# Fetching the expert marks at the start of a round and splitting the gate chain around the w2 splits in a fused attention, mixture-of-experts and dense kernel

## The reference

```python
def _moe_ref(x, expert_emb, tau, w1, w2):
    N, D = x.shape                                   # 4608, 512
    xn = x / (np.linalg.norm(x, axis=-1, keepdims=True) + 1e-06)
    en = expert_emb / (np.linalg.norm(expert_emb, axis=-1, keepdims=True) + 1e-06)
    logits = xn @ en.T / tau
    expert_idx = np.argmax(logits, axis=1)
    logits_shift = logits - logits.max(-1, keepdims=True)
    probs = np.exp(logits_shift)
    probs /= probs.sum(-1, keepdims=True) + 1e-09
    gate_w = probs[np.arange(N), expert_idx]
    for e in range(E):                               # E = 8
        mask = expert_idx == e
        h = np.maximum(x[mask] @ w1[e], 0.0)         # w1: 512 x 1024
        out[mask] = gate_w[mask, None] * (h @ w2[e]) # w2: 1024 x 512
    return out

def _moe2_ref(x, w_in, w_out, s, b):
    h = x @ w_in                                     # 512 x 2048
    g = s * np.maximum(h, 0.0) ** 2 + b
    return g @ w_out                                 # 2048 x 512
```

## Time and profile before

| What | Value |
|---|---|
| Median of three executions | 1391.1 us (1390.35 to 1391.83) |
| The profiled execution, its own time | 1393.17 us |
| Its span, first to last instruction | 1391.1 us |
| TensorE busy | 1345.2 us, 97% of the span |
| VectorE busy | 645.1 us, 46% |
| ScalarE busy | 506.7 us, 36% |
| GpSimd busy | 192.6 us, 14% |
| Mean granted TensorE clock | 0.993 of full speed |

### The profile page before, as it was taken

How to read it: one execution, slowest core, us unless ns; L and a number is a source line. 1 busy time by engine, 2 the same in 40 slices (tenths; PEclk the granted TensorE clock), 3 DMA queues, 4 the chain that set the end, 5 groups by cost and what they waited for, 6 DMA issues and landing times.

```text
span 1391.1 us, 23074 instructions
## 1 busy us (share of the span) xinstructions
PE 1345.2 (97%) x6908; PEld 1105.3 (79%) x6909; DVE 645.1 (46%) x1648; ACT 506.7 (36%) x951; POOL 192.6 (14%) x341
## 2 busy tenths in 40 slices
PE   7998899999999999999999999999999999999996
PEld 5776688877788778779888888888888888888884
DVE  5898546666645664757323223232232332322322
ACT  4885335545434643544222222222222222222221
POOL 2236322221222122200001001000010010100101
PEclk9999999999999999999999999999999999999998
DMA  8755313553512451240100001001010010100000
GB/s 252 224 145 193 115 57 103 180 184 108 184 49 68 149 185 49 71 170 9 48 0 31 32 0 62 0 15 47 0 62 0 0 62 0 62 0 0 31 0 31
DMA packets 71938, 103.61 MB, mean 74 GB/s; under 512 B 40424, under 2 KB 41048, under 8 KB 70624
## 3 DMA queue, kind: packets, MB, share of 16 engines
q1 hardware_dynamic: 57824, 72.16, 15.8%
q0 software_dynamic: 8448, 20.40, 4.4%
q10 hardware_dynamic: 5632, 10.60, 2.0%
HBM read 71.81 MB, written 31.34 MB: 74 GB/s over the span
## 4 chain that ended last, share of the span: by engine, by line
PE 81%; DVE 7%; issue 4%; DMA 2%; DVEq 2%; POOL 1%; ACT 1%; ACTq 0%; POOLq 0%; SPq 0%
PE bank_a L1570 26%; PE bank_n L1589 14%; PE bank_tt L1589 12%; PE bank_a L1492 11%; PE bank_n L1525 10%; DMA xg<-x_tok,g_idx 2%; PE bank_tt L1505 1%; PE bank_n L1423 1%; DVEq L363 1%; POOL slot_tab L497 1%; PE bank_tt L1294 1%; PE bank_a L1275 1%; DVE w_in_lo L1044 1%; DVEq L366 1%; PE bank_l L1556 1%
## 5 line engine op out<-in xcount | busy, mean ns | idle before, releaser
L1212 DVE TENSOR_TENSOR sq<-rel 128x512 f32<-128x512 f32 (+1 forms) x144 | 95.4, 663 | 478.4 <-ACT rel L817 478.4
L817 ACT ACTIVATE rel<-bank_a 128x512 f32<-128x512 f32 (+1 forms) x144 | 82.8, 575 | 534.9 <-PE bank_a L1570 534.9
L1570 PE MATMUL bank_a<-y_hi,w_in_hi 128*128 128x512 f32 (+1 forms) x576 | 218.1, 379 | 1.5 <-DVE y_lo L1204 1.4
L1570 PE MATMUL bank_a<-y_hi,w_in_lo 128*128 128x512 f32 (+1 forms) x576 | 217.6, 378 | 0.0
L1570 PE MATMUL bank_a<-y_lo,w_in_hi 128*128 128x512 f32 (+1 forms) x576 | 217.6, 378 | 0.0
L582 POOL DMA_INDIRECT out_rows<-w_raw,out_id x34 | 32.9, 968 | 714.5 <-DVE w_raw L1223 652.1
L1570 PEld LDWEIGHTS bank_a<-y_hi,w_in_hi 128*128 128x128 f32 x576 | 108.4, 188 | 23.0 <-DVE y_lo L1204 1.8
L1570 PEld LDWEIGHTS bank_a<-y_lo,w_in_hi 128*128 128x128 f32 x576 | 108.4, 188 | 20.6 <-issue 0.2
L1570 PEld LDWEIGHTS bank_a<-y_hi,w_in_lo 128*128 128x128 f32 x576 | 108.4, 188 | 19.9
L1525 PE MATMUL bank_n<-w_hi,hid_hi 128*128 128x512 f32 x296 | 115.5, 390 | 1.5 <-DVE hid_lo L1069 1.5
L1525 PE MATMUL bank_n<-w_hi,hid_lo 128*128 128x512 f32 x296 | 115.4, 390 | 0.0
(11 more groups left out here) (237 smaller groups left out, 2136.3 us busy)
## 6 DMA issues: line engine op xcount, KB each, us to landing
w_raw<-in_moe_w SPq DMA_DIRECT2D x16, 2048.0 KB, 10.6
moe_tok<-yg ACTq DMA_DIRECT2D x38, 272.0 KB, 2.1
x_tok<-x_rows SPq DMA_DIRECT2D x8, 1088.0 KB
y_rows<-moe_tok SPq DMA_DIRECT2D x8, 1088.0 KB, 5.3
x_m<-in_x SPq DMA_DIRECT2D x7, 1024.0 KB, 9.4
win_raw<-in_moe_w_in SPq DMA_DIRECT2D x8, 512.0 KB, 10.7
w_raw<-in_moe_w_out SPq DMA_DIRECT2D x1, 4096.0 KB, 16.2
slot_tab<-w_lo SPq DMA_DIRECT2D x2, 1152.0 KB, 6.6
```

What stands on the lines that cost most here:

```text
L817: nc.scalar.activation(rel[:, k, 0:cols], ps_g[k][:, 0:cols], ACT.Relu).then_inc(rel_ready, 1)
L1212: nc.vector.tensor_tensor(sq[:, 0:cols], rel[:, k, 0:cols], rel[:, k, 0:cols], ALU.mult).then_inc(sq_ready, 1)
L1570: last = nc.tensor.matmul(ps_g[n % 2][:, 0:cols], w[:, wc], a[:, c, 0:cols], start=(c == 0 and w is w_in_hi and a is y_hi), stop=(c == DC ...
```

## The change

The table gets one more entry, the last tile less one, and each engine reads it. In a round, VectorE and ScalarE read the marks of tiles g and g+1 (ScalarE the output row too) at the round's start, and `next_w1`, `next_w2` and `store` take them as arguments. On VectorE, `gate_scale` is cut into `gate_norm` (8 steps) and `gate_root` (9 steps), with `next_w2` between them. On ScalarE, `next_w2` comes before `store`. The loop ends one round earlier on TensorE, VectorE, ScalarE and GpSimd, and the last round is written out with only the work that the last tile needs.

```diff
@@ gpsimd
-            with pool.Fori(2, last) as g:
+            with pool.Fori(2, prev) as g:
                 gather(g + 3)
                 result_ids(g)
+            result_ids(prev)
             result_ids(last)
@@ scalar
-            def store(g):
+            def store(g, row=None):
+                row = rows_of(act, g) if row is None else row
                 act.wait_ge(yg_ready, g + 1)
                 act.wait_ge(yid_done, g + 2)
-                act.dma_start(moe_tok[ds(rows_of(act, g), P), :], yg[:]).then_inc(moe_stored, 16)
+                act.dma_start(moe_tok[ds(row, P), :], yg[:]).then_inc(moe_stored, 16)
...
             def tile(g):
+                e, changes = experts(g)
+                e_next, changes_next = experts(g + 1)
+                row = rows_of(act, g)
                 hidden(g + 1)
                 x_hi(g + 2)
                 gate_square(g + 3)
-                next_w1(g + 1)
+                next_w1(e_next, changes_next)
                 gate_soft(g + 1)
                 result(g)
                 hidden_hi(g + 1)
-                store(g)
-                next_w2(g)
-
-            with act.Fori(2, last) as g:
+                next_w2(e, changes, e_next)
+                store(g, row)
+
+            with act.Fori(2, prev) as g:
                 tile(g)
+            hidden(last)
+            gate_soft(last)
+            result(prev)
+            hidden_hi(last)
+            e_a, c_a = experts(prev)
+            e_b, _ = experts(last)
+            next_w2(e_a, c_a, e_b)
+            store(prev)
@@ vector
+            def experts(g):
+                return expert_of(dve, g), changes_after(dve, g)
...
+            def gate_norm(g):
+                n_gate, gate_link = gate_linker(g, 0)
                 dve.wait_ge(gate_lg, g + 1)
...
+                rsqrt_seed(gate_link, gc[:, 0:1], gc[:, 4:5].bitcast(i32), gi[:, 0:1])
+                rsqrt_rounds(gate_link, gc[:, 4:5], gc[:, 5:6], gc[:, 0:1], 1)
+                assert n_gate[0] == NORM_STEPS
+
+            def gate_root(g):
+                n_gate, gate_link = gate_linker(g, NORM_STEPS)
+                rsqrt_rounds(gate_link, gc[:, 4:5], gc[:, 5:6], gc[:, 0:1], 2)
                 gate_link(nc.vector.tensor_tensor(gc[:, 6:7], gc[:, 0:1], gc[:, 4:5], ALU.mult))
                 gate_link(nc.vector.tensor_scalar(gc[:, 6:7], gc[:, 6:7], NORM_EPS, None, ALU.add))
                 nc.vector.reciprocal(gc[:, 1:2], gc[:, 6:7]).then_inc(gate_in, 1)
...
             def tile(g):
+                e, changes = experts(g)
+                e_next, changes_next = experts(g + 1)
                 x_lo(g + 2)
                 gate_logits(g + 3)
-                next_w1(g + 1)
+                next_w1(e_next, changes_next)
                 gate_final(g + 1)
                 hidden_lo(g + 1)
-                gate_scale(g + 2)
-                next_w2(g)
-
-            with dve.Fori(2, last) as g:
+                gate_norm(g + 2)
+                dve.sem_inc(norm_turn, 1)
+                next_w2(e, changes, e_next)
+                gate_root(g + 2)
+
+            with dve.Fori(2, prev) as g:
                 tile(g)
+            gate_final(last)
+            hidden_lo(last)
+            e_a, c_a = experts(prev)
+            e_b, _ = experts(last)
+            next_w2(e_a, c_a, e_b)
@@ tensor
-            with pe.Fori(2, last_g) as g:
+            prev = tile_ahead_of_last(pe)
+            with pe.Fori(2, prev) as g:
                 tile(g)
+            turn_hidden(prev)
+            up(last_g)
+            down(prev)
             turn_hidden(last_g)
```

More of the change, by code:

```diff
@@ L86, in attention_moe_ffn @@
         emb_t = sb(top, "emb_t", [P, PAIRS, E], f32)
-        tile_tab = sb(top, "tile_tab", [P, 3 * NSLOT + 1], i32)
+        tile_tab = sb(top, "tile_tab", [P, 3 * NSLOT + 2], i32)
         slot_w = sb(top, "slot_w", [P, IDW], f32)
@@ L99, in attention_moe_ffn @@
         gi = sb(top, "gi", [P, 2], i32)
-        used = sum(-(-n // 32) * 32 for n in (4 * P, 4 * P, 2 * P, 2 * P, 4 * PAIRS * E, 4 * (3 * NSLOT + 1), 4 * IDW, 4, 4 * NSLOT, 4 * NSLOT,
+        used = sum(-(-n // 32) * 32 for n in (4 * P, 4 * P, 2 * P, 2 * P, 4 * PAIRS * E, 4 * (3 * NSLOT + 2), 4 * IDW, 4, 4 * NSLOT, 4 * NSLOT,
                                               4, 4, 4, 4 * TROWS, 4 * E, 4 * E, 32, 8))
@@ L163, in attention_moe_ffn @@
         tab_f = sb(am, "tab_f", [P, 4, NSLOT], f32)
-        tab_o = sb(am, "tab_o", [P, 3 * NSLOT + 1], f32)
+        tab_o = sb(am, "tab_o", [P, 3 * NSLOT + 2], f32)
         o_slot = sb(am, "o_slot", [P, NSLOT], f32)
@@ L177, in attention_moe_ffn @@
             4 * COLS, 2 * COLS * E, 4 * E, 2 * (B + 1) * E, 4 * COLS, 4 * B * COLS, 4 * COLS * E, 4 * COLS * E, 4 * B * COLS * IDW,
[L178 removed]
+            4 * NSLOT, 8 * E, 48 * E, 4 * NSLOT * E, 4 * NSLOT * E, 16 * NSLOT, 4 * (3 * NSLOT + 2), 4 * NSLOT, 4, 4 * NSLOT, 16, 4 * E,
             4 * E, 4 * NSLOT, 4 * NSLOT * E, 4 * NSLOT, 4 * RW))
@@ L316, in attention_moe_ffn @@
         gate_in = sem("gate_in")
+        norm_turn = sem("norm_turn")
         gate_exp = sem("gate_exp")
@@ L347, in attention_moe_ffn @@
         GATE_STEPS = 17
+        NORM_STEPS = 8
         O_C = TROWS - HEAD
@@ L360, in last_tile, with tile_ahead_of_last @@
             return eng.value_load(tile_tab[0:1, 3 * NSLOT:3 * NSLOT + 1], min_val=E - 1 + EARLY - 1, max_val=MAXT - 1)
+        def tile_ahead_of_last(eng):
+            return eng.value_load(tile_tab[0:1, 3 * NSLOT + 1:3 * NSLOT + 2], min_val=E - 1 + EARLY - 2, max_val=MAXT - 2)
         def expert_of(eng, g):
@@ L443, in _ @@
             sp.sem_inc(load_turn, 1)
-            sp.wait_ge(gate_sq, last + 3)
+            sp.wait_ge(gate_sq, last + 2)
             sp.sem_inc(load_turn, 1)
@@ L548, in _ @@
             last = last_tile(pool)
+            prev = tile_ahead_of_last(pool)
             def result_ids(g):
@@ L701, in win_hi, with next_w1 @@
                 nc.scalar.activation(w_in_hi[:, ds(e * SLOT, SLOT)], win_raw[:], ACT.Copy).then_inc(win_hi_done, 1)
-            def next_w1(g):
-                e = expert_of(act, g)
-                with act.If(changes_after(act, g) > 0):
+            def experts(g):
+                return expert_of(act, g), changes_after(act, g)
+            def next_w1(e, changes):
+                with act.If(changes > 0):
                     act.wait_ge(w1_loaded, 16 * e + 32)
@@ L709, in next_w1, with next_w2 @@
                         nc.scalar.activation(w1_hi[:, c], w_raw[:, c], ACT.Copy).then_inc(w1_hi_done, 1)
-            def next_w2(g):
-                e = expert_of(act, g)
-                with act.If(changes_after(act, g) > 0):
+            def next_w2(e, changes, e_next):
+                with act.If(changes > 0):
                     act.wait_ge(w2_loaded, 16 * e + 32)
@@ L717, in next_w2 @@
                                              w_raw[:, WCOLS + k * SLOT:WCOLS + (k + 1) * SLOT], ACT.Copy).then_inc(w2_hi_done, 1)
-                    win_hi(expert_of(act, g + 1))
+                    win_hi(e_next)
             def hidden_hi(g):
@@ L759, in _ @@
             act.wait_ge(tab_ready, 1)
-            next_w1(1)
+            next_w1(*experts(1))
             act.wait_ge(st_stored, 16 * B)
@@ L771, in _ @@
             x_hi(3)
-            next_w1(2)
+            next_w1(*experts(2))
             hidden_hi(2)
@@ L776, in _ @@
             gate_soft(2)
-            next_w2(1)
+            e_a, c_a = experts(1)
+            e_b, _ = experts(2)
+            next_w2(e_a, c_a, e_b)
             last = last_tile(act)
+            prev = tile_ahead_of_last(act)
             def tile(g):
+                e, changes = experts(g)
+                e_next, changes_next = experts(g + 1)
+                row = rows_of(act, g)
                 hidden(g + 1)
@@ L848, in emb_link, with rsqrt_seed, rsqrt_rounds @@
                 dve.wait_ge(emb_step, n_emb[0])
-            def rsqrt_steps(link, y, t, n2, iy, it):
+            def rsqrt_seed(link, n2, iy, it):
                 link(nc.vector.tensor_single_scalar(it, n2.bitcast(i32), 1, ALU.arith_shift_right))
                 link(nc.vector.tensor_scalar(iy, it, -1.0, RSQRT_SEED, ALU.mult, ALU.add))
-                for _ in range(3):
+            def rsqrt_rounds(link, y, t, n2, rounds):
+                for _ in range(rounds):
                     link(nc.vector.scalar_tensor_tensor(t, y, n2, y, ALU.mult, ALU.mult))
@@ L873, in embed @@
                 emb_link(nc.vector.reciprocal(inv_tau[:], inv_tau[:]))
-                rsqrt_steps(emb_link, en[0:E, 1:2], en[0:E, 2:3], en[0:E, 0:1], en[0:E, 1:2].bitcast(i32), ei[0:E, 0:1])
+                rsqrt_seed(emb_link, en[0:E, 0:1], en[0:E, 1:2].bitcast(i32), ei[0:E, 0:1])
+                rsqrt_rounds(emb_link, en[0:E, 1:2], en[0:E, 2:3], en[0:E, 0:1], 3)
                 emb_link(nc.vector.tensor_tensor(en[0:E, 3:4], en[0:E, 0:1], en[0:E, 1:2], ALU.mult))
@@ L1045, in win_lo, with experts, next_w1 @@
                     .then_inc(win_ready, 1)
```

(37 more changed lines are left out.)

1 line of the change is left out of this document (removed).

## The result

The changed kernel takes 1413.72 us (median of four executions, 1412.77 to 1417.44) against 1391.46 us: a ratio of 1.0166, 95% interval 1.0145 to 1.0186. It is 22.3 us slower. The forecast was 1418.3 us, range 1394 to 1428. The profiled execution took 1414.42 us, its span is 1412.2 us, 21.1 more than before, and its mean granted clock 0.986 (before 0.993).

What follows compares the result with a forecast made beforehand. TensorE, with 81% of the chain, was taken as the bound, stalling in seven expert-change rounds. Late `x_lo` +14.7, clock +15.0, last round −2.0 and two −0.25 terms gave +27.2 on 1391.1: 1418.3 us, range 1394 to 1428.

Steps and rivals of the forecast that it cites:

- Splits earlier: Expert-change rounds: w2 splits start 3.0 us earlier, so TensorE's `down` no longer waits for them.
- `x_lo` later: Seven expert-change rounds: `x_lo` waits for root half, loop end and four marks; 2.1 us each, +14.7 us.
- The clock: TensorE's longer gap at expert changes halves the granted clock in six of seven, 2.5 us each: +15.0 us.
- Common rounds: Rounds without expert change: `x_lo` comes 1.35 us later, but 0.7 us is left, so nothing is lost.
- The last round: Written-out last tile: `turn_x` goes, `y_lo` comes earlier, the dense stage's 1.39 us of idleness goes: −2.0 us.
- Ahead of the loop: Before the loop: `store(0)` reads its row before its wait, less GpSimd's extra load: −0.25 us.
- The faster one: Rival: loop end and marks are hidden, `x_lo` starts 0.75 us earlier than before, clock holds: 1383.3 us; chance 0.16.
- Loads that overlap: Rival: before `x_lo`, four mark loads cost 1.95 us as two do, clock up: 1394.2 us; chance 0.08.
- The clock that holds: Rival: `x_lo` is late at expert changes but TensorE's clock stays up: 1403.3 us; chance 0.22.

Runs made afterwards that it cites:

- e1: Changed kernel with VectorE's root half moved behind the next round's `x_lo`: 1391.09 us against 1405.68 for the kernel before, ratio 0.9909.
- e2: Changed kernel with VectorE's marks loaded right ahead of the branches as before, root half still behind the w2 splits: ratio 1.0038 to the kernel before.
- e3: Changed kernel with VectorE's gate chain whole and ahead of the w2 splits, marks still at the round's start: ratio 0.9901 to the kernel before.
- e8: The changed kernel unedited, run again beside the kernel before on the same chip: ratio 1.0165 to the kernel before.
- e4: Changed kernel with twelve unused constant matmuls ahead of `turn_x` where TensorE waits for the late `x_lo`: 1416.05 us against 1405.68 before, ratio 1.0086.
- e5: Changed kernel with VectorE's round as before; ScalarE's part, table and written-out last round stay changed: ratio 0.9966 to the kernel before.
- e7: The kernel before, unedited, profiled again on the chip of a later set: loop (`up(3)` to last `up`) 429.54 us.

## Why the prediction was right, point by point

- **Splits earlier, that half of the stall gone: right.** 3.0 us earlier was the sum; from the start of `hidden_lo` to the splits it was 236.75 − 230.47 = 6.28 and is 232.04 − 228.66 = 3.38, 2.9 less. The store's DMA left at 228.80, 0.2 us before the first copy started, so costing it at nothing was right.
- **`x_lo` later: right, and the main cause** (e1, e2, e3). 3.30 us were to lie behind the root half's end; the wait is 3.17. So 2.1 us a round became 1.96: seven times gives 13.7, not 14.7. That the 2 us need both the early marks and the root half ahead of them is shown by e2 on one side and by e3 and e1 on the other.
- **The clock: right in kind and count, too dear.** Six of seven fell, as taken; but a fall cost 1.85 us on the mean, not 2.5, so 11.1 us and not 15.0. This is the mis-sized term of the sum. The step that failed is the price, taken for all six from the one fall of before, 6.8 us long. Three of the six were as long and cost 2.30 to 2.48 us, near the 2.5. The other three came later, after `turn_x` had started, lasted 3.4 us and cost 1.25 to 1.35. One of these (TensorE, then a stretch as in the earlier trace rows):

```profile
286.56 0.63 PE L1477 MATMUL bank_n<-ident,xg 128*128 128x128 f32 x4 [3.18 <-DVE xg_lo L1000]
```

```profile
287.10:290.50 3.40, 3.02 (x8) 2.35 (x8) 2.58 (x11) 0.00 (x0) 1.73 (x3) 0.50 0.92 337
```

In e8 two falls were long (2.2 and 2.5 us) and five short (1.0 to 1.6). What decides between long and short no run shows. That six was the right count is luck in part: there was one fall to go by, and the same kernel had seven in e8. That the falls cost this and are not a mere sign is shown by e4. The Trainium skill (TensorE: Matmul & The Clock Gate, "What's actually happening") has the half rate as the default that activity lifts; the twelve matmuls of e4, whose result nobody reads, kept the rate up, which agrees.
- **Common rounds: partly wrong.** "0.7 us is left, so nothing is lost" missed two things. In the loop's first round the loads of the table's last entries and of four marks stand right behind a whole gate chain, so `x_lo` comes 4.15 us behind it; that round takes 13.2 us, +1.0. Without the early marks (e2, e5) or with the root half moved (e1) it takes 12.2 to 12.3, so the new entry alone does not cost it. And in the rounds ahead of four of the long ones `up` starts about 0.1 us late, +0.5 in all.
- **The last round:** −2.4 where −2.0 was said, a little outside its bounds. The 1.39 us are gone; half a microsecond more went behind it.
- **Ahead of the loop:** −0.25 was said, −2.8 came, of which 1.9 is a fall of the clock in the profile of before. That the profile I worked from had an event in it that the other executions lack I could not see from one execution.
- **The total.** The medians differ by 22.3 us and the profiles by 21.1, where +27.2 was forecast. The two losses in the sum were 4.9 us too high and the gains at both ends 3.0 too small; the 1.5 us lost in common rounds, put at nothing, hid part of that by luck.
- **The rivals.** The faster one needed less than 1.14 us between root half and `x_lo`; it is 3.17. Loads that overlap: four took 2.7 us in a row, no overlap. The clock that holds: at one of the seven gaps, and at all seven only when work is put in them (e4).

## What to carry to other kernels

An engine's sequencer can hide register loads, branches and waits under its own long instructions, but only as far as the next wait for a result of its own engine (the same four marks cost no idle time in e3 and 3.17 us with the loop's end in the changed kernel). Put chains of small dependent steps behind the thing that others wait for, and never between long work and a load-heavy loop head. Two edits of which one is good alone (marks early) and one costs little (chain split) can be bad together (with neither the ratio is 0.997, with the one 0.990, with the other 1.004, with both 1.017), so try them apart. And when TensorE is made to wait longer, count the rounds behind the wait too: here the clock took nearly as much again as the wait.

## What the runs showed of the hardware that I had not expected

- The clock falls at shorter gaps than I had expected, and not each time. In e2 TensorE is idle for 1.75 us before `turn_x`, and the clock fell at five of the seven changes; in the kernel before the same places had 0.2 us of idleness and none fell in two profiles. With gaps of 3.0 to 3.2 us it fell at six of seven, and in e8 at all seven. Ahead of the loop each of the two profiles of the kernel before has one fall, but at different places (154.4 and 129.3 us).
- The stretch ahead of the loop differs from set to set while the loop does not: `up(3)` starts at 168.9 us in the first profile of before and at 174.4 in e7, and the loops differ by 0.3 us. Already `up(0)`, behind the attention, starts at 124.9 and 131.5. What makes it so was not looked into; it is why only ratios within a set were used.
